# GpSimd's share of a fused attention and MLP kernel: the order within a slot changed, and a wait ahead of each instruction

## The reference

```python
scores = scale * q @ k.T                      # per head, 576 x 576
cum    = cumsum(max(s, 0))
scores = where(causal, -1e9, scores + min(-(cum_i - cum_j), 0))
attn   = softmax(scores);  x = attn @ v       # -> x: 2304 x 512
h = x @ w_in;   y = (h - tanh(h)) @ w_out     # 512 -> 2048 -> 512
h = y @ w2_in;  h = h * softmax(h);  h = layernorm(h) * g;  out = h @ w2_out
```

## Time and profile before

| | |
|---|---|
| median of 3 executions | 812.92 us (812.18 to 813.12) |
| the profiled execution's own time | 813.12 us |
| its span in the profile | 811.3 us |
| attention (from the start to the first product with w_out) | 0 to 217 us |
| busy PE, DVE, ACT, POOL | 98%, 57%, 49%, 34% of the span |

### The profile page before, as it was taken

The page is one execution under the profiler, slowest core; times in us unless marked ns, Lnnn a source line. Parts: engine busy times, 40 slices in busy tenths (PEclk is TensorE's granted clock), DMA queues, the critical chain, the costliest instruction groups (busy, mean ns, idle before and its releaser), DMA issues. The chain is left out here.

```text
span 811.3 us, 14584 instructions
## 1 busy us (share of the span) xinstructions
PE 796.5 (98%) x4498; PEld 669.9 (83%) x4498; DVE 465.4 (57%) x1101; ACT 396.0 (49%) x935; POOL 273.1 (34%) x322
## 2 busy tenths in 40 slices
PE   6999999998999999999999999999999999999998
PEld 5888888887888899988888888888887788888886
DVE  5888998898854332332233222453568666666661
ACT  4999999998543332322232222542434344443342
POOL 4678778877100000000000000016553754444400
PEclk9999999999999999999999999999999999999999
DMA  7565555544433200000000000002000000000001
GB/s 186 138 161 155 138 157 160 147 118 146 133 116 104 78 1 1 1 1 1 0 1 0 0 0 0 1 0 100 5 0 1 27 26 27 27 20 19 23 16 52
DMA packets 77722, 46.39 MB, mean 57 GB/s; under 512 B 59824, under 2 KB 68144, under 8 KB 77680
## 3 DMA queue, kind: packets, MB, share of 16 engines
q1 hardware_dynamic: 75232, 45.19, 19.4%
q10 hardware_dynamic: 2448, 0.66, 0.4%
HBM read 40.97 MB, written 4.87 MB: 56 GB/s over the span
## 5 line engine op out<-in xcount | busy, mean ns | idle before, releaser
L1458 PE MATMUL psum<-x_hi,w1i 128*128 128x512 f32 (+1 forms) x640 | 181.9, 369 | 0.0
L1471 PE MATMUL psum<-gate_hi,w1o 128*128 128x512 f32 (+1 forms) x640 | 146.0, 370 | 0.0
L1458 PEld LDWEIGHTS psum<-x_hi,w1i 128*128 128x128 f32 x640 | 115.5, 188 | 20.6 <-DVE w1i L1111 0.4
L1471 PEld LDWEIGHTS psum<-gate_hi,w1o 128*128 128x128 f32 x640 | 112.4, 188 | 21.1
L1154 DVE TENSOR_TENSOR gate_lo<-gate,gate_hi 128x512 fp32r<-128x512 f32 (+1 forms) x80 | 53.6, 670 | 125.0 <-ACT gate_hi L861 125.0
L1458 PE MATMUL psum<-x_lo,w1i 128*128 128x512 f32 (+1 forms) x320 | 117.7, 368 | 0.0
L703 POOL TENSOR_TENSOR w2t<-stage 128x512 f32<-128x512 f32 x2 | 4.3, 2154 | 328.0 <-DVE w2x L1128 328.0
L861 ACT ACTIVATE gate_hi<-gate 128x512 fp32r<-128x512 f32 (+1 forms) x80 | 47.2, 590 | 134.7 <-PE psum L1471 126.5
L1142 DVE TENSOR_TENSOR gate<-psum,gate 128x512 f32<-128x512 f32 (+1 forms) x80 | 51.0, 638 | 95.9 <-ACT gate L848 94.3
L848 ACT ACTIVATE gate<-psum 128x512 f32<-128x512 f32 (+1 forms) x80 | 44.4, 555 | 111.8 <-PE psum L1458 90.8
L886 ACT ACTIVATE probs<-probs,neg_max 128x128 f32<-128x128 f32 (+2 forms) x144 | 83.5, 586 | 10.0 <-DVE neg_max L1187 9.7
(11 more groups left out here) (154 smaller groups left out, 1408.3 us busy)
## 6 DMA issues: line engine op xcount, KB each, us to landing
cum_bc<-cum_dram SPq DMA_DIRECT2D x16, 576.0 KB, 4.6
rden_T<-rden_dram SPq DMA_DIRECT2D x32, 144.0 KB, 3.1
out_x<-out_sb SPq DMA_DIRECT2D x18, 256.0 KB, 2.0
stage<-in_q SPq DMA_DIRECT2D x32, 128.0 KB, 2.4
v_raw<-in_v SPq DMA_DIRECT2D x32, 128.0 KB, 3.6
stage<-in_moe_w_in SPq DMA_DIRECT2D x16, 256.0 KB, 2.8
stage<-in_moe_w_out SPq DMA_DIRECT2D x16, 256.0 KB, 3.1
stage<-in_k SPq DMA_DIRECT2D x28, 128.0 KB, 2.4
```

The lines of the kernel that those rows point to most:

```text
L1458: mm = pe.matmul(h_ps[j % 4][:, 0:wide(c)], wp[j][:, kt, :], xp[:, kt, 0:wide(c)], start=(n == 0), stop=(n == 3 * KT - 1))
L1471: mm = pe.matmul(y_ps[m][:, 0:wide(c)], wp[j][:, m * P:(m + 1) * P], gp[j % 2][:, 0:wide(c)], start=(j == 0 and wp is w1o_hi and gp is gat ...
```

## The change

Three things change, all of them in GpSimd's stream and all inside a slot. First, `scale_x` moves ahead of `v_hi`, and `v_hi` and `v_lo` become one function `split_v` that comes last. Second, each of GpSimd's instructions in a slot now waits for a semaphore that the one before it raises when it is complete. Third, one wait that stood ahead of the second copy of `cum_tail` moves ahead of the first, so that the first copy waits for the previous slot's `v_lo`. No arithmetic, no buffer and no other engine's stream is changed.

```diff
                         wait(pool, biased, TILES * pair)
+                        wait(pool, v_split, 2 * pair)
                         met(pool)
                         pool.tensor_copy(cum_tail[0:TAIL, :], ...).then_inc(cum_copied, 1)
-                        wait(pool, v_split, 2 * pair)
+                        pool.wait_ge(cum_copied, 2 * pair + 1)
                         met(pool)
                         pool.tensor_copy(cum_tail[TAIL:P, :], ...).then_inc(cum_copied, 1)
...
                         if n == 0:
                             pool.wait_ge(cum_copied, 2 * (pair - 1) + 2)
+                        else:
+                            pool.wait_ge(qk_lo, 3 * pair + n)
                         met(pool)
                         pool.tensor_copy(hi, flat).then_inc(qk_hi, 1)
...
                         pool.wait_ge(rden_in[par], 32 * (half + 1))
+                        if sl.runs(1):
+                            pool.wait_ge(qk_lo, 3 * sl.pair(1)[0] + 3)
+                        elif sl.runs(0):
+                            pool.wait_ge(cum_copied, 2 * sl.pair(0)[0] + 2)
+                        else:
+                            pool.wait_ge(x_done, pair)
                         pool.wait_ge(x_added, 2 * pair + 2)
                         met(pool)
                         pool.tensor_tensor(dst, x_sum[:, :], rden_T[par][:, :], ALU.mult).then_inc(x_done, 1)
...
-                def v_hi():
+                def split_v():
                         pool.wait_ge(v_in[par], 48 * (half + 1))
+                        pool.wait_ge(cum_copied, 2 * pair + 2)
+                        if sl.runs(1) and not (sl.fixed and sl.s <= 0):
+                            pool.wait_ge(qk_lo, 3 * sl.pair(1)[0] + 3)
+                        wait(pool, x_done, pair - 1)
                         wait(pool, attended, 2 * (pair - 1))
-                        pool.wait_ge(cum_copied, 2 * pair + 2)
                         met(pool)
-                        pool.tensor_copy(high(v_parts[par]), v_raw[par]...).then_inc(v_split, 1)
+                        pool.tensor_copy(high(v_parts[par]), raw).then_inc(v_split, 1)
                         pool.wait_ge(v_split, 2 * pair + 1)
                         met(pool)
                         pool.tensor_tensor(low(v_parts[par]), raw, ...).then_inc(v_split, 1)
...
                     for kt in tiles:
                         pool.wait_ge(cum_copied, 2 * PAIRS)
+                        wait(pool, x_lo_done, kt)
...
                 if sl.fixed and sl.s == PAIRS - 1:
                     first_x(0, 1, 2)
+                    pool.wait_ge(x_lo_done, 3)
                 if sl.fixed and sl.s == PAIRS:
                     first_x(3)
-                v_hi()
+                    pool.wait_ge(x_lo_done, 4)
                 scale_x()
-                v_lo()
+                split_v()
```

More of the change, by code:

```diff
@@ L646, in scale_x @@
                         pool.tensor_tensor(dst, x_sum[:, :], rden_T[par][:, :], ALU.mult).then_inc(x_done, 1)
-                def v_hi():
+                def split_v():
                     if sl.runs(0):
                         pair, half, par = sl.pair(0)
+                        raw = v_raw[par].rearrange("p t (h d) -> p t h d", h=2)
                         pool.wait_ge(v_in[par], 48 * (half + 1))
+                        pool.wait_ge(cum_copied, 2 * pair + 2)
+                        if sl.runs(1) and not (sl.fixed and sl.s <= 0):
+                            pool.wait_ge(qk_lo, 3 * sl.pair(1)[0] + 3)
+                        wait(pool, x_done, pair - 1)
                         wait(pool, attended, 2 * (pair - 1))
-                        pool.wait_ge(cum_copied, 2 * pair + 2)
                         met(pool)
[L655 to L659, removed]
+                        pool.tensor_copy(high(v_parts[par]), raw).then_inc(v_split, 1)
                         pool.wait_ge(v_split, 2 * pair + 1)
                         met(pool)
-                        pool.tensor_tensor(low(v_parts[par]), v_raw[par].rearrange("p t (h d) -> p t h d", h=2),
-                                           high(v_parts[par]).bitcast(F32), ALU.subtract).then_inc(v_split, 1)
+                        pool.tensor_tensor(low(v_parts[par]), raw, high(v_parts[par]).bitcast(F32),
+                                           ALU.subtract).then_inc(v_split, 1)
                 def first_x(*tiles):
```

## The result

The changed kernel takes 818.33 us (median of 4, 817.61 to 819.44) against 812.87 us for the kernel before, run beside it (4 executions), a ratio of 1.0077 with a 95% interval of 1.0062 to 1.0090. Run once more beside other kernels its ratio came out the same: 1.0078 (1.0065 to 1.0092), with medians of 819.21 and 812.46 us. Forecast were 816.5 us and a range of 813.4 to 819.8. The direction, the engine and the place were right; the size was 3.6 us where 5.5 were measured.

A forecast was written before the change was run, and what follows sets the result against it. PE sets the loop's 11.77 us slots until GpSimd's round reaches 12.23: ten rounds of 0.46 us make 4.6, less 1.25 of room 3.4, plus 0.2 in the last slots, 3.6 us: 816.5 us, range 813.4 to 819.8.

The forecast's parts named there:

- The waits cost 0.18 us each, the scaling more: GpSimd's eight newly chained boundaries: 0.18 us each, but 0.58 ahead of the loop's scaling and 0.25 ahead of v's cast.
- The new round: GpSimd's loop round: 9.78 us of work plus 2.45 of gaps, 12.23 us against PE's 11.77, so 0.46 lost per round.
- The room: Lag GpSimd can build up before PE's scores or ACT's copy of k run late: 1.25 us for both.
- The order: Scaling ahead of v's cast: DVE's need for the scaling stays hidden by 0.2 to 0.3 us; v's later parts cost nothing.
- Queues: SP's loads that wait for GpSimd's v split or scaling: releases come early enough, cost nothing.
- The last slots: After the loop the lag stands still; DVE waits some 0.2 us for the scaling, the fourth MLP high part just in time.
- Within the room: Rival, 0.20: scaling and v's cast also wait 0.18 us, round 11.76 us, lag never grows: 812.9 us, up to 814.
- A longer chain: Rival, 0.12: register-valued waits cost 0.08 us more at four further boundaries, round 12.55 us, loss 6.5 us: 819.6 us.

The follow-up runs named there:

- the run with the old order: Kernel after with the old order (cast of v, scaling, subtraction of v), every instruction still waiting for the one before: 818.88 us, ratio 1.0084.
- the written-out run: Kernel after with GpSimd's slots all written out with constants, no register arithmetic behind a wait, other engines keeping their loop: 815.89 us, ratio 1.0044.
- the order alone: Kernel before with only the new order (scaling, then cast and subtraction of v), no added wait: 813.99 us, ratio 1.0007.
- the unchained scaling: Kernel after without the scaling's wait for the instruction before it, all other added waits kept: 812.48 us, ratio 0.9999.
- both doses: Kernel before with one more GpSimd memset in each loop slot, large (about 2 us) or half as many columns: 815.43 us (1.0030) and 812.83 us (0.9997).
- the scaling first: Kernel after with slot 15's scaling ahead of the split of the first tokens, loop untouched: 818.51 us, ratio 1.0069.

## Why the prediction was right, and where its sizes were off

*The waits cost 0.18 us each, the scaling more.* Right: 0.16 to 0.18 us at the plain boundaries. The scaling's 0.58 measured 0.64 to 0.67. The queue works from 138.4 to 138.9 in it, on the wait L647 itself, L652, the increment of L356, the address and one more step of L654; which of them makes the difference to my 0.58 isn't shown. The cast of v has 0.35 where I took 0.25, my upper bound: its wait for the scaling is followed by the one for `attended` and by the increment. With constants the scaling needs 0.17, not 0.23, but the cast of v 0.35 and the first copy of `cum_tail` 0.26, so the written-out round is 11.90 and not 11.81 us. One reading of the earlier trace rows was too smooth: the second copy of `cum_tail` starts 0.06 us after the recorded end of the first (127.62 against 127.56), not before it. The sum does not hang on it.

*The new round.* 12.23 forecast, 12.29 to 12.34 measured (12.39 in the last), 12.31 in the middle. Over ten rounds this is 0.8 us more loss.

*The room.* Mis-sized: 1.25 us taken. The last subtraction of k ends 1.01 us before PE's start of slot 4 (1.67 in the kernel before) and 0.13 before the starts from slot 7 on, so 0.88 us were there. The rounds of 11.90 us in the first, written-out slots had used the rest before the loop began. Together the two terms make the loop 4.56 instead of 3.4 us. That both readers, PE at the slot's head and ACT at its copy of k, run out at about the same lag was right: each accounts for half of a slot's loss.

*The order.* "Hidden, by 0.2 to 0.3 us only" held, with less to spare: the sums of DVE start 0.11 to 0.14 us after the scaling ends, which is about what DVE needs to hear of it, and DVE does not idle for it in the loop. "Only thanks to the new order" was right for DVE's wait and wrong for the time, as the run with the old order shows.

*Queues.* No wait of SP in attention ends with GpSimd, in either profile. Its waits for ACT and DVE there did grow, from 13.9 to 16.2 us (`rden_row`) and from 4.0 to 6.5 (`neg_max`), but no wait of PE ends with a load there, and nothing of the 5.73 us is left for it.

*The last slots.* The wait of DVE for the scaling was the right one, 0.53 us instead of 0.2. The lag of k's last subtraction that GpSimd brought from the loop was 1.63 us instead of 1.5, and from its end to the end of the scaling it took 14.06 us (187.65 to 201.71) instead of 13.8. The fourth high part was not quite in time: its cast took 1.07 us instead of 0.61, and in the written-out run, where the clock stayed at 1.00, PE's way from there to the MLP is 2.90 us instead of 2.75. That PE's longer idle time can be followed by a spell at the low clock was missing from the sum. In the two profiles it is worth 1.47 us there and -0.83 us in the first slots. It is a matter of the execution: at this place the profiled executions of the change (twice), of the waits in the old order, of the order alone and of the unchained scaling have it, and those of before, of the written-out slots, of both doses and of the scaling first do not, and both kinds have idle times of 1.2 us and of 1.7 us among them. How much of the difference is the clock can be read from the times of all executions, sorted by their mean granted clock. At a mean of 0.998 the kernel before takes 811.64 to 813.55 us (34 executions, 812.4 on average) and the change 817.61 and 817.73; at 0.996 it is 812.83 to 814.26 (20 executions, 813.8) and 818.81 to 819.14 (7 executions, 819.0). So at an equal clock the change costs 5.2 to 5.3 us, of which the loop's 4.56 and slot 16's 0.53 make 5.1. What is above that in the two comparisons of medians comes with lower clocks: 5 of the change's 14 executions have a mean of 0.994, and none of the 55 of the kernel before is under 0.996.

*The rivals.* "Within the room" failed where it was to decide: the gaps sum to 2.5 us, not 1.99. It came true as soon as the one gap of the scaling was taken out. "A longer chain" named a round of 12.55 us and fell. What the Trainium skill says of the vector engine in "VectorE: DVE Perf Modes", section "The DRAIN you can't avoid", does not carry over to GpSimd: the same instructions start 0.03 to 0.06 us before an end without a wait and 0.16 to 0.18 us after it with one. The Trainium skill has the rule that fits in "GPSIMD Engine Reference", section "2.1 Instruction dispatch": completion holds back what waits on the semaphore, and not the next Pool instruction. The trace agrees.

*What the 0.18 us is made of.* The prediction used 0.08 us for the splits of the first tokens and 0.18 for the others, and did not ask why they differ. Each wait of the loop is followed by `met(pool)`, an increment that is a queue instruction of its own; in `first_x` the wait stands right ahead of the instruction. Two rows of slot 15, after:

```profile
193.87 0.62 POOL L678 CAST x_hi<-xT 128x512 fp32r<-128x512 f32 x1
194.57 1.28 POOL L680 TENSOR_TENSOR x_lo<-xT,x_hi 128x512 fp32r<-128x512 f32 x1
```

The low part waits for the high part here too and starts 0.08 us after its end (193.87 + 0.62 = 194.49). So about 0.1 us of each gap goes with the increment, not with the wait; over the eight new gaps that is an estimated 0.8 us a round, more than the 0.54 us by which the round is too long. No run here leaves the increments out.

## What to carry to other kernels

A serial chain of waits on an engine that looks 34% or 81% busy is free as long as the engine's round, with its gaps, stays below the period of the bounding engine; above that, the excess is paid each round, once the room at the start is used up. So sum one round of the stage and not the page's share. Look at what the queue does behind the blocking wait: an address computed in registers is free while the queue runs ahead and comes onto the path once it can't, and one such wait (0.7 us of 2.5) decided the whole loss here. A wait taken from one place in a chain that is late shows up at the next deadline; look for the latest work, not for the longest wait.

## What the runs showed of the hardware

An instruction of GpSimd that waits for the one before starts 0.16 to 0.18 us after its end, at nine of the eleven boundaries of a round, where one increment stands behind the wait (the other two have more queue work there); without an increment it starts 0.08 us after the end, and without a wait mostly 0.03 to 0.06 us before it. TensorE's granted clock fell to the 1.2 GHz level after idle times of 1.2 to 2.4 us in some executions and not in others; the way from slot 16 to the MLP took 4.08 to 4.35 us with such a spell (five profiled executions) and 2.75 to 2.90 without (five; the run with the scaling first, which has a wait of its own there, is left out). Beside filling two idle moments with products that nobody reads, the kernel's spread narrowed from 3.0 to 1.3 us; a low spell ahead of both places stayed.
